# Gate weights transposed once in device memory, VectorE's products for the logits read contiguous rows and are dealt out 2, 3, 3, 1 to a tile's chunks, and x's high halves are made on ScalarE

## What is computed

```
x    = elu(x @ w_in) @ w_out                      # 2304 x 512, hidden 2048
do   = x @ w_skip > 0
e    = argmax(x @ w_gate)                         # w_gate is 512 x 8
p    = softmax(x @ w_gate)[e]
out  = x + do * p * (relu(x @ w1[e]) @ w2[e])     # 512 -> 1024 -> 512
```

## Time and profile before

| | us |
|---|---|
| median of 3 runs | 862.98 |
| the three runs | 862.17, 862.98, 863.29 |
| the profiled execution, by the same clock | 863.67 |
| its span, first to last instruction | 862.0 |
| busy: PE / DVE / ACT / POOL | 819.0 / 580.3 / 353.6 / 246.2 |
| mean granted TensorE clock, share of full speed | 0.987 |

### The profile page before, as it was taken

The page is one execution under the profiler, slowest core; times in us unless marked ns, Lnnn a source line. Parts: engine busy times, 40 slices in busy tenths (PEclk is TensorE's granted clock), DMA queues, the critical chain, the costliest instruction groups (busy, mean ns, idle before and its releaser), DMA issues.

```text
span 862.0 us, 14995 instructions
## 1 busy us (share of the span) xinstructions
PE 819.0 (95%) x4726; PEld 673.9 (78%) x4727; DVE 580.3 (67%) x1326; ACT 353.6 (41%) x858; POOL 246.2 (29%) x232
## 2 busy tenths in 40 slices
PE   5999999998799999999999999999998899999995
PEld 4777777775799987898898788789886677887884
DVE  4766676766533399779959959963665799376342
ACT  4766766674233322222222232232444387255241
POOL 3656655661344012003012102200011232222121
PEclk9999999999799999999999999999999999999998
DMA  6344444521425202020021020031232499455000
GB/s 146 97 109 120 122 117 109 157 68 54 148 62 161 103 19 68 1 83 19 10 75 28 10 74 0 26 149 48 74 135 79 151 319 338 165 167 188 31 26 8
DMA packets 97489, 83.29 MB, mean 97 GB/s; under 512 B 63452, under 2 KB 74972, under 8 KB 97312
## 3 DMA queue, kind: packets, MB, share of 16 engines
q1 hardware_dynamic: 94384, 77.67, 28.9%
q0 software_dynamic: 3056, 5.00, 1.8%
HBM read 67.54 MB, written 18.25 MB: 100 GB/s over the span
## 4 chain that ended last, share of the span: by engine, by line
PE 48%; DVE 21%; issue 3%; DVEq 1%; ACT 1%; POOL 0%; POOLq 0%; ACTq 0%
DVE x2t L1104 11%; PE h_ps L1540 8%; PE out_ps L1540 8%; PE h_ps L1541 8%; PE h_ps L1542 8%; PE out_ps L1541 7%; PE out_ps L1542 7%; DVE gt L1215 2%; DVE ex L1231 2%; DVE ex L1228 1%; PE out_ps L1669 1%; DVE xt_hi L1222 1%; PE tr_ps L1634 1%; PE lg_ps L1591 1%; DVEq L854 0%
## 5 line engine op out<-in xcount | busy, mean ns | idle before, releaser
L1391 ACT ACTIVATE ex<-h_ps 128x384 f32<-128x384 f32 x96 | 47.4, 493 | 285.0 <-PE h_ps L1542 239.7
L1540 PE MATMUL h_ps<-xt_hi,wi_hi 128*128 128x384 f32 x384 | 133.2, 347 | 5.3 <-DVE xt_lo L1261 5.3
L1541 PE MATMUL h_ps<-xt_lo,wi_hi 128*128 128x384 f32 x384 | 131.2, 342 | 0.0
L1542 PE MATMUL h_ps<-xt_hi,wi_lo 128*128 128x384 f32 x384 | 131.2, 342 | 0.0
L1104 DVE CUSTOM_DVE_ANT_0 x2t<-x,w_raw 128x512 bf16<-128x512 f32 x108 | 129.5, 1244 | 0.4
L1540 PE MATMUL out_ps<-wo_hi,gt 128*128 128x512 f32 x288 | 115.8, 402 | 4.6 <-DVE gt L1215 4.4
L1542 PE MATMUL out_ps<-wo_hi,gt 128*128 128x512 f32 x288 | 113.9, 395 | 0.0
L1541 PE MATMUL out_ps<-wo_lo,gt 128*128 128x512 f32 x288 | 113.4, 394 | 0.0
L1228 DVE TENSOR_SCALAR ex<-ex 128x384 f32<-128x384 f32 x96 | 35.7, 372 | 111.6 <-ACT ex L1391 111.6
L425 ACT ACTIVATE prob<-s_ps,negmax 128x128 f32<-128x128 f32 (+2 forms) x144 | 78.0, 549 | 13.5 <-DVE negmax L305 7.2
L1540 PEld LDWEIGHTS h_ps<-xt_hi,wi_hi 128*128 128x128 f32 x384 | 73.3, 191 | 9.3 <-DVE xt_lo L1261 5.9
(11 more groups left out here) (173 smaller groups left out, 1687.6 us busy)
## 6 DMA issues: line engine op xcount, KB each, us to landing
w_raw<-in_moe_w_dram SPq DMA_DIRECT2D x56, 512.0 KB, 5.7
attn_t<-attn_sb SPq DMA_DIRECT2D x16, 288.0 KB, 2.2
x_raw<-attn_t SPq DMA_DIRECT2D x24, 192.0 KB, 2.4
out_dram<-x SPq DMA_DIRECT2D x18, 256.0 KB, 2.5
x_rows<-x SPq DMA_DIRECT2D x18, 256.0 KB, 2.8
raw_qk<-in_q_dram SPq DMA_DIRECT2D x32, 128.0 KB, 2.5
raw_qk<-in_k_dram SPq DMA_DIRECT2D x32, 128.0 KB, 2.5
v<-in_v_dram SPq DMA_DIRECT2D x32, 128.0 KB, 2.4
```

Of the source, the lines that this page charges most:

```text
L1391: act.activation(ex[:, f % 2], h_ps[:, f % 2, 0:NB], ACT.Exp).then_inc(ex_done, 1)
L1540: pe.matmul(dst, stat[0], mov[0], start=start, stop=False, skip_group_check=True)
L1541: pe.matmul(dst, stat[0], mov[1], start=False, stop=False, skip_group_check=True)
L1542: return pe.matmul(dst, stat[1], mov[0], start=False, stop=stop, skip_group_check=True)
```

## The change

- A scratch tensor `gates_t` of 8 x 512 in device memory. Behind the fourth w_out slice and the x rows of block 1, SP issues a DMA that copies w_gate into it transposed, element by element, before the slice of chunk 4.
- `broadcast_gates` waits for that copy and reads `gates_t`; `all_gates` is `[8, 512]` in each partition, so that each product reads a contiguous row.
- The nine products of a tile are dealt out 2, 3, 3, 1 in place of 3, 2, 2, 2.
- `x_hi` for blocks 1 to 5 moves from DVE's step to ACT's, behind `g_hi` of the same step. Block 0's stays on DVE.

```
-        all_gates = w1_raw[:, :, :, :].rearrange("p j o f -> p (j o f)").rearrange("p (d e) -> p d e", e=E)
+        all_gates = w1_raw[:, :, :, :].rearrange("p j o f -> p (j o f)").rearrange("p (e d) -> p e d", e=E)
+        gates_t = nc.dram_tensor("gates_t", (E, DM), F32, kind="Internal").ap()
...
             def broadcast_gates():
-                sp.dma_start(all_gates.rearrange("p d e -> p (d e)"),
-                             w_gate.rearrange("(o d) e -> o (d e)", o=1).broadcast_to([P, DM * E]))\
+                sp.wait_ge(gates_turned, 16)
+                sp.dma_start(all_gates.rearrange("p e d -> p (e d)"),
+                             gates_t.rearrange("(o e) d -> o (e d)", o=1).broadcast_to([P, DM * E]))\
                   .then_inc(all_gates_in, 16)
...
             for f in range(FC):
+                if f == WR:
+                    sp.dma_start(gates_t, w_gate.rearrange("d e -> e d"), allow_slow_non_contiguous=True)\
+                      .then_inc(gates_turned, 16)
                 wait(sp, wo_lo_done, f - WR + 1)
...
-                    ins = dve.tensor_tensor_reduce(..., x2[s][:, :], all_skip if e == E else all_gates[:, :, e],
+                    ins = dve.tensor_tensor_reduce(..., x2[s][:, :], all_skip if e == E else all_gates[:, e, :],
...
-            def x_hi(b, k):                                   # DVE
-                dve.wait_ge(xr_in[k], 16 * (b + 1))
-                if k == 0:
-                    wait(dve, h_done, FC * (b - 1))
-                dve.tensor_copy(xtk(b % 2, 0, k), x_raw[k][:, :]).then_inc(x_hi_done, 1)
...
-                if f in X_AT and b < LAST:
-                    x_hi(b + 1, X_AT.index(f))
...
-                        dots(b - 1, s, ((0, 1, 2), (3, 4), (5, 6), (7, 8))[f - DOT_AT(s)])
+                        dots(b - 1, s, ((0, 1), (2, 3, 4), (5, 6, 7), (8,))[f - DOT_AT(s)])
...
+            def x_hi(b, k):                                   # ACT
+                act.wait_ge(xr_in[k], 16 * (b + 1))
+                if k == 0:
+                    wait(act, h_done, FC * (b - 1))
+                if b == 1 and k == 0:
+                    act.wait_ge(x_hi_done, KC)
+                act.activation(xtk(b % 2, 0, k), x_raw[k][:, :], ACT.Copy).then_inc(x_hi_done, 1)
...
+                if f in X_AT and b < LAST:                    # ACT's step, behind g_hi
+                    x_hi(b + 1, X_AT.index(f))
```

More of the change, by code:

```diff
@@ L783, in experts @@
         all_gates_in = sem("all_gates_in")
+        gates_turned = sem("gates_turned")
         table_init = sem("table_init")
@@ L1103, in dots @@
                     wait(dve, dot_done, E * t + e - 1 if e > 1 else E * t)
-                    ins = dve.tensor_tensor_reduce(dot_rows[:, ((E + 1) * t + e) % 2], x2[s][:, :], all_skip if e == E else all_gates[:, :, e],
+                    ins = dve.tensor_tensor_reduce(dot_rows[:, ((E + 1) * t + e) % 2], x2[s][:, :], all_skip if e == E else all_gates[:, e, :],
                                                    1.0, 0.0, ALU.mult, ALU.add, logits_sb[t % 2][:, e:e + 1])
@@ L1258, in _ @@
             for k in range(KC):
-                x_hi(0, k)
+                dve.wait_ge(xr_in[k], 16)
+                dve.tensor_copy(xtk(0, 0, k), x_raw[k][:, :]).then_inc(x_hi_done, 1)
                 dve.wait_ge(x_hi_done, k + 1)
```

## The result

882.62 us is the median of the changed kernel, 863.13 that of the kernel before in the same runs: a ratio of 1.0223, 95% interval 1.0206 to 1.0241. The change is slower by 19.5 us; 851.0 was forecast. The profiled execution took 883.1 us, span 881.4.

A forecast was written before the change was run, and what follows sets the result against it. PE, 95% busy, bounds the kernel, with late DVE chunks costing it 12.05 us in the four `dots` blocks; `x_hi` and the copy cost nothing. 862.98 - 12.05 = 850.9, forecast 851.0 us, range 850.0 to 861.5.

The forecast's parts named there:

- I take N about 11, so a cost of nothing: Block 0: the transposing copy delays w_out slices of chunks 4 to 7 by its length N, about 11 us, hidden.
- my upper end of 24.3: Copy's length in us at w_skip's mean rate if its eight rows use only eight engines.
- All four estimates: Copy's length from w_skip's 512 four-byte pieces: 5.1 us dense rate, 12.2 mean; doubled on eight engines, 10.2 and 24.3.
- its bound of 300 ns: Upper price per small write to device memory, from `route_table`'s 128 eight-byte pieces in 2.4 us, 8 to an engine.
- The rival that came true: Copy in block 0: each 4-byte write to device memory is dear; at 60 ns, 868.5 us; chance 0.15.
- the other late-slice rival: Block 0: eight rows on eight engines at mean rate, copy 24.3 us, PE stalls 9.6, total 862.1; chance 0.20.
- The free 14.7 us: Block 0: chunk 4's w_out slice may land at 241.2 instead of about 226.5 before PE is held up.
- The clock's price after a gap: PE after an idle stretch runs near 1.2 GHz; about 1.6 us lost.
- 12.05 us to gain in blocks 1 to 4: Blocks with `dots`: DVE lateness costs PE 282.72 against a floor of 270.67 us; all of it to be gained.
- Products 0.68: DVE's 96 changed gate products take 0.68 us each with contiguous rows, against 1.17.
- The collision: DVE product running beside POOL's `x_lo`: 0.81 us more for a strided one; contiguous, between nothing and 1.30.
- `x_hi` on ACT cost nothing: ACT, blocks 1 to 5: 20 copies of 0.52 us, 10.4 in all, hidden in ACT's idle time.

The follow-up runs named there:

- the bench: Kernel before plus only the transposing copy to device memory, result unread; 894.91 us with writes 4 bytes apart, 887.76 at 8, 870.51 at 32.

## Why the prediction was wrong

- **The step that failed** is the term "I take N about 11, so a cost of nothing". N was 42.2 us, beyond even my upper end of 24.3. All four estimates were scaled from w_skip's load, which writes to SBUF; the pieces of this copy follow one another in device memory. The run into SBUF shows that the row was right for what it showed (7.5 us, between the 5.1 and the 10.2 of the dense rate) and the wrong row for this target. I had named that doubt in the rival, and had left its bound of 300 ns out of the range.
- **The rival that came true** is the slower one, given 0.15: at 60 ns a piece it said 868.5; the price was 42.2 / 512 = 82 ns and the time 882.6; with N at 42.2 its own sum gives 850.9 + 27.5 + 1.6 = 880.0. Its reason was half right: not each small write to memory is dear, but one that lies close to others. The condition of the other late-slice rival, eight engines for eight rows, was true as well; its 24.3 us fell short because its rate came from the same row.
- The free 14.7 us were about right. The gap by that rule would be 42.2 - 14.7 = 27.5; 31.72 were measured. The layer had started 2.8 us earlier, and from the landing to PE it took 272.50 - 268.90 = 3.6, not 2.44; with both the rule gives 31.5.
- The clock's price after a gap was put at 1.6 us from the earlier trace rows; here 2.7.
- **Right:** 12.05 us to gain in blocks 1 to 4; 11.89 came. Products 0.68; 0.686 at the median. The collision was bounded by 0 and 1.30; the longest product, 1.506, is 0.83 over an undisturbed one. (The sum had two collisions a block; the trace has four, in the first block at 340.1, 348.5, 357.1 and 365.5. DVE had room for them.) `x_hi` on ACT cost nothing, nor did its wait. PE was next to bound, without a gap.
- **Credited too widely:** I gave the 12 us to three edits together. The contiguous rows alone bring it all, and the other two nothing on top of them that these runs show; without the rows those two bring 1.5 us.

## What to carry to other kernels

A one-time preparation moved into a queue is priced by what it makes late, and its length belongs in the range at the widest end that the rows allow: here one 16 KB copy of 4096 pieces held up loads that had 14.7 us to spare for 42. When a DMA must move small pieces, send them to SBUF, or spread them in device memory, or at least walk them so that neighbours don't follow one another, and give it an outer dimension that all 16 engines can share; the one try at another issuing queue made it worse. Where an engine was over its budget in lumps, shortening the dear operation brought the gain; dealing it out anew did little.

## What was not expected of the hardware

Four-byte writes 4 bytes apart in device memory made the load behind them late by 81 ns for each of an engine's 512 pieces, those 64 bytes apart by 19, those to SBUF by 15. And SP did not get free of the next load: its issue, 0.43 us in the earlier trace rows, took 31.59 behind the copy, 30.48 in the bench at 4 bytes, 25.03 at 8 and 10.79 at 32. So small pieces that move slowly also hold up the engine that feeds the queue.
